# Attention queries transposed raw with each head's row doubled, their high and low parts made behind the transpose, and half of GpSimd's weight splits put behind a wait for a pair's masks

## The reference

```python
scores = scale * (q @ k^T)                # 2 batches, 8 heads, 576 x 64
keep the 32 largest scores of each row, softmax over them, attn = P @ v
x = attn as (1152, 512)
x = mixture of 8 experts: relu(x @ w1[e]) @ w2[e], gates by 8 rounds of row and column normalising
x = (h * tanh(softplus(h))) @ w_out, h = x @ w_in
```

## Time and profile before

| | us |
|---|---|
| median of 3 runs (range) | 1239.48 (1239.37 to 1240.28) |
| the profiled execution, whole | 1242.88 |
| its span | 1241.0 |
| PE busy | 1198.6 (97%) |
| DVE busy | 899.6 (72%) |
| ACT busy | 687.6 (55%) |
| POOL busy | 642.6 (52%) |

### The profile page before, as it was taken

The page is one execution under the profiler, slowest core; times in us unless marked ns, Lnnn a source line. Parts: engine busy times, 40 slices in busy tenths (PEclk is TensorE's granted clock), DMA queues, the critical chain, the costliest instruction groups (busy, mean ns, idle before and its releaser), DMA issues.

```text
span 1241.0 us, 19573 instructions
## 1 busy us (share of the span) xinstructions
PE 1198.6 (97%) x6676; PEld 1071.3 (86%) x6676; DVE 899.6 (72%) x1556; ACT 687.6 (55%) x1226; POOL 642.6 (52%) x393
## 2 busy tenths in 40 slices
PE   4878999999999999999999999999999999999998
PEld 4777889999999998999888999999888888898777
DVE  6989998899999971446646564646464647887886
ACT  5666776767777664442243333333333337888776
POOL 1857965555656567763376666666666630000000
PEclk8599999999999999999999999999999999999999
DMA  9023432233323233332233222222222122222230
GB/s 170 9 86 120 144 104 93 94 94 107 110 90 111 86 111 102 120 102 93 85 106 107 69 75 76 75 80 74 86 67 94 52 68 85 69 69 84 86 125 36
DMA packets 150486, 112.10 MB, mean 90 GB/s; under 512 B 34832, under 2 KB 124944, under 8 KB 150416
## 3 DMA queue, kind: packets, MB, share of 16 engines
q1 hardware_dynamic: 150416, 111.19, 29.6%
HBM read 104.09 MB, written 7.08 MB: 90 GB/s over the span
## 4 chain that ended last, share of the span: by engine, by line
PE 86%; DVE 7%; ACT 3%; POOL 2%; issue 2%; DMA 1%; SPq 0%; ACTq 0%; DVEq 0%; POOLq 0%
PE ps L903 16%; PE ps L728 15%; PE ps L741 15%; PE ps L964 14%; PE ps L1031 7%; PE ps L1087 7%; PE ps L637 4%; PE ps L608 3%; DVE top L1486 2%; DVE work L1488 2%; PE ps L618 2%; PE ps L597 1%; POOL s_sb L1961 1%; PE ps L632 1%; POOL e_sb L1964 1%
## 5 line engine op out<-in xcount | busy, mean ns | idle before, releaser
L1890 POOL TENSOR_TENSOR w_lo<-w_raw,w_hi 128x1024 fp32r<-128x1024 f32 x90 | 219.6, 2440 | 114.4 <-ACT w_hi L1114 114.3
L1114 ACT ACTIVATE w_hi<-w_raw 128x1024 fp32r<-128x1024 f32 (+1 forms) x172 | 179.4, 1044 | 0.6 <-DMA w_raw<-in_k 0.6
L1486 DVE MAX8 top<-work 128x8 f32<-128x576 f32 x216 | 152.3, 747 | 0.0
L728 PE MATMUL ps<-x_hi,w_hi 128*128 128x384 f32 (+3 forms) x384 | 128.2, 334 | 0.1
L728 PE MATMUL ps<-x_hi,w_lo 128*128 128x384 f32 (+3 forms) x384 | 127.4, 332 | 0.0
L728 PE MATMUL ps<-x_lo,w_hi 128*128 128x384 f32 (+3 forms) x384 | 127.2, 331 | 0.0
L1897 POOL TENSOR_TENSOR ha_lo<-h_f,ha_hi 128x384 fp32r<-128x384 f32 (+1 forms) x72 | 72.0, 999 | 90.4 <-ACT ha_hi L1191 90.4
L903 PE MATMUL ps<-w_hi,h_lo 128*128 128x512 f32 x296 | 117.1, 396 | 0.0
L903 PE MATMUL ps<-w_lo,h_hi 128*128 128x512 f32 x296 | 116.9, 395 | 0.0
L903 PE MATMUL ps<-w_hi,h_hi 128*128 128x512 f32 x296 | 115.3, 390 | 0.0
L1488 DVE MATCH_REPLACE8 work<-top,work 128x576 f32<-128x576 f32 x144 | 105.9, 743 | 0.0
(11 more groups left out here) (185 smaller groups left out, 3273.1 us busy)
## 6 DMA issues: line engine op xcount, KB each, us to landing
w_raw<-in_moe_w SPq DMA_DIRECT2D x288, 256.0 KB, 3.0
w_raw<-in_moe_w_in SPq DMA_DIRECT2D x32, 256.0 KB, 2.8
w_raw<-in_moe_w_out SPq DMA_DIRECT2D x32, 256.0 KB, 3.1
spill<-y_out SPq DMA_DIRECT2D x5, 768.0 KB, 3.8
y_in<-spill SPq DMA_DIRECT2D x5, 768.0 KB, 4.4
q_parts<-in_q SPq DMA_DIRECT2D x18, 128.0 KB, 3.3
vones<-in_v SPq DMA_DIRECT2D x8, 256.0 KB, 4.9
out<-acc SPq DMA_DIRECT2D x8, 256.0 KB, 2.7
```

The source lines that it names most:

```text
L728: last = nc.tensor.matmul(ps[:, bank, 0:w], wt[:, s, 0, c * P:(c + 1) * P], xt[:, c, token:token + w], start=(n == 0), stop=(n == len(term ...
L1114: return nc.scalar.activation(dst, src, ACT.Copy)
L1486: last = v_.max(top[:, b, op // 2, :], src)
L1890: g_.tensor_tensor(w_lo[:, s, :, :].rearrange("p a n -> p (a n)"), w_raw[:, s, :, :].rearrange("p a n -> p (a n)"), w_hi[:, s, :, :].rearr ...
```

## The change

Queries are loaded twice, beside each other, into `q_raw` (128 rows, 8 heads, 2 copies, 64 columns). A transpose of one head's 128 columns then gives the head's raw queries twice, one above the other. There are two rounds g of four transposes for a tile instead of four: round 0 of tile T+1 in step 5 of tile T, round 1 of tile T+1 in its own step 1. From PSUM ACT copies a round to `q_f` (float32) and again, rounded, to the high half of `q_s`; POOL subtracts and writes the low half. In tile 0 there is no `q_f` and DVE subtracts, reading PSUM. `q_s` now holds (high, high) and (low, low) instead of (high, low) and (low, high); with (high, low) of the keys below each other the four part products are the same. `queries_high` is gone. PE waits for the load itself before a round, and for POOL's `q_low` before the scores of heads 0 and 4.

POOL's list gets a subtraction for each round, at hand-written places in tiles 0 to 3; and in `tile_with_chunks` the weight split of steps 0, 2, 4 and 6 comes after `pair_done`, a wait until the two masks of the pair that PE transposes in this step and the next are on.

```diff
-        q_parts = sb("q_parts", [P, H, 3, D], F32R, where=early)
+        q_raw = sb("q_raw", [P, H, 2, D], where=early)
+        q_f = sb("q_f", [P, H // 2, P], where=early)
...
+            def load_queries(*places):
+                for n, (b, start) in enumerate(places):
+                    rows = P // len(places)
+                    for a in range(2):
+                        sp.dma_start(q_raw[n * rows:(n + 1) * rows, :, a, :],
+                                     q_v[b, bass.ds(start, rows)]).then_inc(q_in, 16)
...
-            def queries_transposed(T, r):
+            def queries_transposed(T, g):
+                pe.wait_ge(q_in, 16 * queries_in(T))
                 for i in range(HH):
-                    last = nc.tensor.transpose(ps[:, query_bank(T, r), i * P:(i + 1) * P],
-                                               q_parts[:, r // 2 * HH + i, r % 2:r % 2 + 2, :].bitcast(F32).rearrange(
-                                                   "p a d -> p (a d)"), ident[:, :])
+                    last = nc.tensor.transpose(ps[:, query_bank(T, g), i * P:(i + 1) * P],
+                                               q_raw[:, g * HH + i, :, :].rearrange("p a d -> p (a d)"), ident[:, :])
                 last.then_inc(q_tr, 1)
...
-            def queries_high(T):
-                act.wait_ge(q_in, 32 * T + 32)
-                copy(q_parts[:, :, 0, :], raw_queries())
-                copy(q_parts[:, :, 2, :], raw_queries()).then_inc(q_high, 1)
...
+            def queries_copied(T, g):
+                act.wait_ge(q_tr, 2 * T + g + 1)
+                at = ps[:, query_bank(T, g), :].rearrange("p (h n) -> p h n", h=HH)
+                if not isinstance(T, int) or T > 0:
+                    act.wait_ge(q_low, 2 * T + g)
+                    copy(q_f[:, :, :], at)
+                copy(queries_of(g, 0), at).then_inc(q_copied, 1)
...
-            first_queries_low()
-            for c in range(3):
-                keys_low(c)
+            keys_low(0)
+            first_queries_low(0)
+            keys_low(1)
+            first_queries_low(1)
+            keys_low(2)
...
+            def queries_low(T, g):
+                pool.wait_ge(q_copied, 2 * T + g + 1)
+                g_.tensor_tensor(queries_of(g, 1), q_f[:, :, :], queries_of(g, 0), ALU.subtract).then_inc(q_low, 1)
...
+            def pair_done(T, h):
+                late = T - 1 if h < 4 else T
+                pool.wait_ge(topk, topk_value(late, (h - 4) % H + 1, MASKED))
...
-                    chunk_a(*chunk_at(T, h))
-                    if h == 3 and following:
-                        queries_low(T + 1)
+                    expert, f = chunk_at(T, h)
+                    hidden_low(expert, f)
+                    if h == 1:
+                        queries_low(T, 1)
+                    if h == 5 and following:
+                        queries_low(T + 1, 0)
+                    if h % 2 == 0:
+                        pair_done(T, h)
+                    split_lo(A0 + expert * NF + f + AHEAD, (f + AHEAD) % RING)
...
             mask(0, 0)
             mask(0, 1)
-            queries_low(1)
+            queries_low(1, 0)
             mask(0, 2)
             mask(0, 3)
...
             keys_low(2)
+            queries_low(1, 1)
             keys_low(3)
             mask(0, 6)
...
             mask(1, 1)
-            queries_low(2)
+            queries_low(2, 0)
...
-            for h in range(4, H):
-                mask(1, h)
+            mask(1, 4)
+            mask(1, 5)
+            queries_low(2, 1)
+            mask(1, 6)
+            mask(1, 7)
             normalised(1, 0)
             normalised(1, 1)
             mask(2, 1)
-            queries_low(3)
+            queries_low(3, 0)
             split_lo(0, 0)
             x_low(1)
             split_lo(1, 1)
...
             hidden_low(*chunk_at(3, 1))
+            queries_low(3, 1)
             mask(2, 7)
...
             chunk_a(*chunk_at(3, 3))
-            queries_low(MIX)
             hidden_low(*chunk_at(3, 4))
             x_low(2)
             split_lo(9, 1)
-            for h in range(LAG, H):
+            chunk_a(*chunk_at(3, LAG))
+            queries_low(MIX, 0)
+            for h in range(LAG + 1, H):
```

More of the change, by code:

```diff
@@ L282, in build, with queries_of @@
         KEYS_FIRST, KEYS_0, KEYS_1 = KC - 2, 2 * KC - 2, 4 * KC - 2
-        def raw_queries(rows=slice(0, P)):
-            return q_parts[rows, :, 1, :].bitcast(F32)
+        def queries_of(g, part):
+            return q_s[:, part, g * HH:(g + 1) * HH, :]
         def x_bank(T):
@@ L291, in build, with queries_in, query_bank @@
         V_LOADS = TB + 2
+        def queries_in(T):
+            return 2 * T + 2 if isinstance(T, int) and T < MIX else 2 * T + 4
         def rest_values(b, rows, a):
             return vones[rows * REST:(rows + 1) * REST, b, TB, :, :].rearrange("p (g a) d -> p g a d", a=2)[:, :, a, :]
-        def query_bank(T, r):
-            return (PT_BANK, O_BANK, 7, 6)[r] if isinstance(T, int) and T == 0 else PT_BANK
+        def query_bank(T, g):
+            return (PT_BANK, O_BANK)[g] if isinstance(T, int) and T == 0 else PT_BANK
         A0, BC0 = -NF, (NA - 1) * NF
@@ L490, in load_ahead, with next_queries @@
                         spill_out(e)
[L492 to L496, removed]
+            def next_queries(T, *places):
+                sp.wait_ge(q_tr, 2 * T)
+                load_queries(*places)
+            load_queries((0, 0))
             for c in range(KC):
@@ L661, in tile_body @@
                     expert, f = chunk_at(T, h)
-                    if h in (1, 2) and not first:
-                        pe.wait_ge(q_copied, 4 * T + h + 2)
-                    if h in (6, 7) and following:
-                        pe.wait_ge(q_copied, 4 * T + h - 1)
+                    if h == 2 and not first:
+                        pe.wait_ge(q_copied, 2 * T + 2)
+                    if h == 6 and following:
+                        pe.wait_ge(q_copied, 2 * T + 3)
+                    if h == 0:
+                        pe.wait_ge(q_low, 2 * T + 1)
+                    if h == 4:
+                        pe.wait_ge(q_low, 2 * T + 2)
                     if first and h == 4:
-                        pe.wait_ge(q_copied, 4)
                         pe.wait_ge(k_copied, KEYS_0)
@@ L675, in tile_body @@
                         up_a(expert, f)
-                    if h in (0, 1) and not first:
+                    if h == 1 and not first:
                         pe.wait_ge(pt_copied, head(T - 1, h + 4) + 1 + FREE)
-                        queries_transposed(T, h + 2)
-                    if h in (5, 6) and following:
+                        queries_transposed(T, 1)
+                    if h == 5 and following:
                         pe.wait_ge(pt_copied, head(T, h - 4) + 1 + FREE)
-                        pe.wait_ge(q_low, T + 1)
-                        queries_transposed(T + 1, h - 5)
+                        queries_transposed(T + 1, 0)
                     if first and h == 4:
@@ L1125, in keys_copied @@
                 copy(key_place(b, c, g), key_columns(c, KEY_BANKS[b, g][c])).then_inc(k_copied, 1)
-            def queries_high(T):
-                act.wait_ge(q_in, 32 * T + 32)
-                copy(q_parts[:, :, 0, :], raw_queries())
-                copy(q_parts[:, :, 2, :], raw_queries()).then_inc(q_high, 1)
-            def queries_copied(T, r):
-                act.wait_ge(q_tr, 4 * T + r + 1)
-                copy(q_s[:, r % 2, r // 2 * HH:(r // 2 + 1) * HH, :].rearrange("p a n -> p (a n)"),
-                     ps[:, query_bank(T, r), :]).then_inc(q_copied, 1)
+            def queries_copied(T, g):
[5 more added lines that the diff above has]
+                copy(queries_of(g, 0), at).then_inc(q_copied, 1)
             def scores_copied(T, h, reused=True):
@@ L1229, in tile_body @@
                         hidden_a(expert, f)
-                    if h in (0, 1) and not first:
-                        queries_copied(T, h + 2)
-                    if h in (5, 6) and following:
-                        queries_copied(T + 1, h - 5)
+                    if h == 1 and not first:
+                        queries_copied(T, 1)
+                    if h == 5 and following:
+                        queries_copied(T + 1, 0)
                     if late_on:
                         output_copied(late, (h - 4) % H, two_before if h < 4 else before)
-                    if h == (4 if first else 3) and following:
-                        queries_high(T + 1)
                     if not early and h == H - 1:
```

39 lines of the change are left out of this document (12 added, 27 removed).

## The result

The changed kernel takes 1254.66 us (median of 4 runs, 1252.49 to 1256.08), the kernel before 1239.42 us (median of 4, 1239.22 to 1240.28): a ratio of 1.0117, with a 95% interval of 1.0106 to 1.0129. I had forecast slower, at 1245.2 us and at most 1250. The direction was right; the size was not. (The ratio is not that of the two medians, which divide to 1.0123.)

A forecast was written before the change was run, and what follows sets the result against it. PE bounds the kernel from about 164 us to attention's end; before, DVE's selection, POOL's masks and PE with ACT's copies feed each other. +1.2 + 2.4 + 2.4 + 4.1 - 4.4 = +5.7 us: 1245.2 us, range 1238.5 to 1250.

The forecast's parts named there:

- Dropped rounds, tiles 4 to 8: Where PE is full, each tile loses two rounds of four: 10 rounds of 0.44 us, -4.4 us, at least 3.5 saved.
- The wait for the masks: Tiles 4 to 8: POOL's wait for the pair's masks is met on arrival, costing and bringing nothing.
- rival 4: Mask wait works and DVE paces the full stretch: shorter masks, same 4.4 us, losses made up in tile 4; 1243; chance 0.03.
- Head: Kernel start: doubled query load and DVE's two subtractions delay first scores by 1.2 us, bounds 0.5 and 1.8.
- Tile 0, POOL's list: Query subtractions wait for PE's round and ACT's copies, delaying masks and tile 1's row sums: +2.4 us, bounds 1.0 and 3.5.
- Tile 1 to 2: `queries_low(2, 1)` ahead of head 6's mask delays masks and row sums: +2.4 us, bounds 2.0 and 2.6.
- Tile 2 to 3: `queries_low(3, 0)` waits for ACT's copies, delaying splits, low part of x and masks: +4.1 us, bounds 2.0 and 5.5.
- rival 3: Much slower: PE idles longer in tiles 2 and 3, the granted clock falls, time passes 1250 with high bounds; chance 0.06.
- Profiled against median: Whole kernel: the profiled execution's 3.4 us above the median was taken off, giving 1245.2 instead of 1248.6 us.
- The signs that I had named: POOL idle before `queries_low`; row-sum waits at least 3.8, 0.5, 1.4 us; first scores 15.2 to 16.5; masks unchanged; repeating tile 50.8.
- Rival 1: Faster: POOL's waits in tiles 0 to 2 are hidden, leaving only the head's +1.2 us; 1236.3 us; chance 0.14.

The follow-up runs named there:

- experiment 4: Changed kernel with the six query subtractions late in POOL's list and DVE's key low parts ahead of query subtractions in the head: 1236.74 us, ratio 0.9972.
- experiment 11: Kernel of experiment 4 with only one of tile 0's two query copies loaded, the other zeros: 1236.71 us, ratio 0.9972.
- experiment 5: Changed kernel with only the two subtractions in tile 0's part of POOL's list moved behind their masks: 1247.38 us, ratio 1.0052.
- experiment 3: Changed kernel without the wait that holds POOL's weight split behind the pair's masks: 1254.69 us, ratio 1.0117.
- experiment 8: Kernel of experiment 4 without the wait that holds POOL's weight split behind the pair's masks: 1236.27 us, ratio 0.9966.
- experiment 1: Changed kernel with POOL's six query subtractions of tiles 0 to 3 moved behind the masks and splits they stood ahead of: 1238.72 us, ratio 0.9988.
- experiment 2: Changed kernel with 28, 16 and 8 unused identity transposes on PE in tile 2, where PE would wait: 1252.43 us, ratio 1.0100.
- 9: Kernel of experiment 4 with identity transposes on PE in tile 0, 30 before the first head's and 6 before each other even head's: 1236.48 us, ratio 0.9969.

## Why the prediction was right in its direction and wrong in its size

- **Dropped rounds, tiles 4 to 8:** right. -4.7 us against -4.4, and -4.2 to -4.7 in all the kernels above. The repeating tile takes 50.9 us, PE full, as forecast.
- **The wait for the masks:** right, no effect (1254.69 against 1254.66, and 1236.27 against 1236.74). The masks keep their length and rival 4 is out.
- **Head:** right in size, +1.5 against +1.2, with luck in the parts. PE's start of the first scores, which is what I had worked out, is 0.95 later. DVE's order costs 1.1 us of it (experiment 4) and the second copy's load 1.3 (experiment 11); I had put the load at 0 to 1.2. So some 1.5 comes back (1.1 + 1.3 - 0.95). ACT's two roundings of queries, which stood ahead of key chunk 0, are the likely place: that chunk is rounded at 6.49 instead of 6.18 although twice the load is ahead of it. I did not try it by itself. The other 0.54 is PE's four scores, 1.30 instead of 0.76 us, and is in no step of mine. 1.31 us is what they take in tile 2 at 137.21, where the granted clock is 0.50 (125.9 to 139.4 us); here the clock column shows 1.00, so the cause isn't shown.
- **Tile 0, POOL's list:** the mechanism is right. Over the five traces that keep tile 0's list the stretch takes 56.8 to 58.4 us, so +1.5 to +3.0 around my +2.4. In the medians, moving it away brings 7.3 us. Where that comes from no trace shows, as the one of experiment 5 is of its slowest execution.
- **Tile 1 to 2:** POOL's wait is right to 0.1 us (31.84 against 31.94). My upper bound of 2.6 is passed because PE's work behind its idle time of 3.35 us runs in part at half clock, 0.62 in the mean: +3.4 us.
- **Tile 2 to 3: the step that failed**, +7.0 against +4.1 with an upper bound of 5.5. I had written that "POOL then runs without gaps, the mask of head 3 ends 4.1 us later". It is 7.1 later. The wait itself I had right: `queries_low(3, 0)` was to end 4.7 us later, and in experiment 3's trace it ends 4.8 later (10.83 us behind the row sums instead of 6.04). What failed is "without gaps". POOL's `hidden_low` ahead of that mask waits for the PE chunk that has itself waited for POOL's `x_low`, so the idle time there does not shrink from 0.69 us to nothing but grows to 1.42, PE doing its part of the circle at half clock; and the split beside a DVE mask takes 0.5 longer. That makes the 6.0 us of experiment 3. The last 1.1 came with the late weight chunk and the half clock behind it, in the changed kernel's trace. Fillers give back 2 us of this stretch.
- **The clock as a rival of its own, at 0.06:** the wrong shape. Its mechanism, as I described it in rival 3, is what happened (0.77 at 120 to 150 us), and so is its time, past 1250. But it was no separate case: it came on top of delays that left PE idle. A lateness of 1.2 us became 4.6 in experiment 8.
- **Profiled against median:** I carried before's 3.4 us over to the changed kernel. Its own profiled execution was on the other side of its median. That is 5.5 of the 9.5 us of error, more than the failed step: with the 9.7 us of the two profiled executions on the median of the kernel before, the time would be 1249.1, within my range. So this was the second step that failed, "it is itself 3.4 above the median" taken off as if the change could not alter it. In medians, putting the six subtractions behind the masks gives back 15.9 us, where my three terms for them add up to 8.9 (a part of the 15.9 is what experiment 1 gains beyond the kernel before). Which stretch holds the rest stays open.
- **The signs that I had named:** POOL idle before `queries_low`, ended by ACT, in tiles 0 to 2 (5.20, 2.93, 4.33, 5.88 us): yes. First scores at 15.2 to 16.5: yes, 15.66. Masks as long as before: yes, 1369 ns in the mean against 1362. The row sums' waits no shorter than 3.8, 0.5 and 1.4 us: 4.13, 3.95, but 0.84 in tile 3, so this sign failed there.
- **The end:** +0.9 us behind the last scores is in no step of mine. Nothing PE, DVE or ACT does is longer there: the last copy ends 2.6 us before the end of the span before, and 3.5 after. All twelve experiments that changed other things show the same 801.4 us; why is open.

Rival 1 (1236.3, all waits hidden) is near what the change is worth with its six subtractions in another place: 1238.7, and 1236.7 with the head in order. That it comes so near is in part luck, since its sum had neither the 0.9 us at the end nor what the new order gains in tiles 0 and 2.

## What to carry to other kernels

When a step of an in-order list starts to depend on other engines, place it again: six lines moved by two or three places were worth 16 us here, and turned a loss of 1.2% into a gain of 0.3% with the next edit. When you price such a wait, look for a circle (does what it delays come back to this same engine?) and for what PE does meanwhile; if PE is left idle, put the half-clock price into the upper bound of that term. Fillers helped where PE was on the path (experiment 2) and not where DVE was (9). One profiled execution may lie several us from its median on either side: before you carry its difference over, see where among the runs of both kernels it stands.

## What the runs showed of the hardware

- **The clock near a gap.** Two executions with the same order of instructions differ by 2.03 against 0.69 us of idle PE at 114 to 116 us, and by a clock of 0.50 against 1.00 from 116.5 to 123. The length of the gap alone does not decide it. In the changed kernel's trace PE idles 2.20 us and goes on at full clock:

```profile
144.05 0.66 PE L627 MATMUL ps<-ident,e_sb 128*128 128x128 f32 x4 [2.20 <-POOL e_sb L1976]
```

There it had idled 2.04 us before the half-clock stretch at 125.91, where four transposes took 1.11. Before the change 2.21 us of idle PE at 130.65 were followed by transposes of 0.63 us. What else must come together is not settled.
- **A late load beside an instruction fetch.** In 4 of 14 profiled executions ACT idled 1.24 to 1.39 us before rounding this weight chunk. The transfers from its issue to the rounding, in the changed kernel:

```profile
GB/s 0 67 0 0 0 0 0 0 67 189 240 219 248 257 345 509 252 307 341 425 320 252 152 118 67 17 0 17 0 17 17 0 17 17 34 0 0 4 29 29
...
q8 instruction: 1, 0.02, 1.6%
```

The bulk is through after two thirds of the 4.9 us; then packets come at some 17 GB/s until the rounding. All four had an instruction fetch of 0.02 MB in that stretch; of the ten without the delay, eight had none and two had one (a smaller one, of 0.01 MB on another queue, stands in 13 of the 14). So it goes with the delay in these 14 traces but is not enough for it. The Trainium skill (Runtime: NRT & Kernel Launch, on instruction fetch mechanics) says that an engine's sequencer fetches its instructions by DMA in blocks of 16 KiB; the row's 0.02 MB agree. Whether the fetch held up the load or ACT's own instructions is not shown.
